# Softmax of the taps on every channel's own row, and two taps of the remaining channels mixed on TensorE, in a two-layer MoE kernel

## What is computed

```python
w = np.exp(weight - weight.max(-1, keepdims=True))          # weight: (8, 7)
w = w / (w.sum(-1, keepdims=True) + 1e-09)
out = np.einsum('hk,bskhg->bshg', w, x_unf)                 # x_unf: 7 shifted copies of x, zeros ahead
h = out @ w_in                                              # layer 1: 192 -> 2048
g = np.where(h >= 1, h, np.where(h <= -1, 0, (h + 1) ** 2 / 4))
x = g @ w_out                                               # 2048 -> 192
r = np.maximum(x @ w_in2, 0)                                # layer 2
return (s * r * r + b) @ w_out2
```

## Time and profile before

| | |
|---|---|
| median of three runs | 1127.93 us |
| the profiled execution's own time | 1127.12 us |
| its span in the profile | 1125.0 us |
| PE busy | 1117.5 us (99%) |
| DVE busy | 857.4 us (76%) |
| ACT busy | 692.0 us (62%) |
| POOL busy | 3.5 us |

### The profile page before, as it was taken

How to read it: one execution, slowest core, us unless ns; L and a number is a source line. 1 busy time by engine, 2 the same in 40 slices (tenths; PEclk the granted TensorE clock), 3 DMA queues, 4 the chain that set the end, 5 groups by cost and what they waited for, 6 DMA issues and landing times.

```text
span 1125.0 us, 22920 instructions
## 1 busy us (share of the span) xinstructions
PE 1117.5 (99%) x9756; PEld 981.5 (87%) x9756; DVE 857.4 (76%) x775; ACT 692.0 (62%) x690; POOL 3.5 (0%) x16
## 2 busy tenths in 40 slices
PE   8999999999999999999999999999999999999998
PEld 6888888888888888888888888888888888888887
DVE  7998888687787777877788677787777877666665
ACT  6977765576555756556655666556655566665544
POOL 1000000000000000000000000000000000000000
PEclk9999999999999999999999999999999999999999
DMA  5121100100000000010000100001000000000000
GB/s 159 30 67 52 44 1 1 29 29 1 1 1 29 29 1 1 1 29 29 1 1 1 40 18 1 1 11 47 1 1 1 1 29 1 1 1 1 29 1 29
DMA packets 13044, 21.30 MB, mean 19 GB/s; under 512 B 1184, under 2 KB 5792, under 8 KB 12960
## 3 DMA queue, kind: packets, MB, share of 16 engines
q1 hardware_dynamic: 12800, 19.86, 6.1%
q10 hardware_dynamic: 96, 0.13, 0.0%
q0 software_dynamic: 64, 0.00, 0.0%
HBM read 13.70 MB, written 6.29 MB: 18 GB/s over the span
## 4 chain that ended last, share of the span: by engine, by line
PE 98%; DVE 1%; DMA 0%; ACT 0%; issue 0%; ACTq 0%
PE h L821 31%; PE acc L868 30%; PE acc_rem L879 20%; PE h L834 15%; PE acc L1019 1%; DMA stage<-in_moe_w_out 0%; DVE mixed_rem L652 0%; PE h L1002 0%; PE acc L908 0%; ACT shared L540 0%; DVE g L558 0%; DVE up_lo L682 0%; ACT g_hi L370 0%; PE acc_rem L902 0%; DVE x_rem L752 0%
## 5 line engine op out<-in xcount | busy, mean ns | idle before, releaser
L561 DVE SCALAR_TENSOR_TENSOR g<-r,scale,h 128x1024 f32<-128x1024 f32 x128 | 161.8, 1277 | 95.1 <-ACT r L351 95.0
L372 ACT ACTIVATE g_hi<-g,shift 128x1024 fp32r<-128x1024 f32 x127 | 146.4, 1153 | 114.3 <-PE acc_rem L879 104.9
L348 ACT ACTIVATE r<-h,half 128x1024 f32<-128x1024 f32 x128 | 138.0, 1112 | 115.5 <-PE h L834 115.0
L351 ACT ACTIVATE r<-h 128x1024 f32<-128x1024 f32 x128 | 127.4, 1026 | 127.2 <-PE h L834 123.7
L821 PE MATMUL h<-x_rem,up_rem_hi 64*128 64x512 f32 x1016 | 204.7, 386 | 0.0
L868 PE MATMUL acc<-g_hi,dn_hi 64*128 64x512 f32 x1016 | 204.6, 386 | 0.0
L879 PE MATMUL acc_rem<-g_lo,dn_rem 64*128 64x512 f32 x1016 | 204.6, 386 | 0.0
L879 PE MATMUL acc_rem<-g_hi,dn_rem 64*128 64x512 f32 x1016 | 204.6, 386 | 0.0
L868 PE MATMUL acc<-g_lo,dn_hi 64*128 64x512 f32 x1016 | 204.6, 386 | 0.0
L868 PE MATMUL acc<-g_hi,dn_lo 64*128 64x512 f32 x1016 | 204.6, 386 | 0.0
L582 DVE SCALAR_TENSOR_TENSOR g_lo<-g,shift,g_hi 128x1024 fp32r<-128x1024 f32 x127 | 162.7, 1281 | 34.9 <-ACT g_hi L372 34.9
(11 more groups left out here) (152 smaller groups left out, 1406.9 us busy)
## 6 DMA issues: line engine op xcount, KB each, us to landing
xraw<-in_x SPq DMA_DIRECT2D x7, 518.0 KB, 4.2
out<-res SPq DMA_DIRECT2D x7, 512.0 KB, 3.3
stage<-in_moe_w_out SPq DMA_DIRECT2D x6, 384.0 KB, 3.3
xraw_rem<-in_x SPq DMA_DIRECT2D x14, 129.5 KB, 3.9
out<-res_rem SPq DMA_DIRECT2D x7, 256.0 KB, 3.7
stage<-in_moe_w_in SPq DMA_DIRECT2D x6, 256.0 KB, 5.8
stage<-in_moe_w_in SPq DMA_DIRECT2D x2, 512.0 KB, 4.7
xraw<-in_x SPq DMA_DIRECT2D x2, 256.0 KB, 2.9
```

The source lines that it names most:

```text
L348: nc.scalar.activation(r[k][:], h[k][:], ACT.Relu, scale=0.5, bias=half[:, 0:1]).then_inc(r_ready if two else relu_done[k], 1)
L351: nc.scalar.activation(r[k][:], h[k][:], ACT.Relu).then_inc(r_ready, 1)
L372: nc.scalar.activation(dst[:], g[k][:], ACT.Identity, bias=shift[:, 0:1]).then_inc(hi_ready, 1)
L561: nc.vector.scalar_tensor_tensor(g[k][:], r[k][:], scale[:, 0:1], h[k][:], ALU.mult, ALU.mult).then_inc(h_used, 1)
```

## The change

The 8-row load, the matrix `head_of` and the three spreading matmuls go. In their place:

- `head_rows` cuts the channels at head borders. ScalarE issues two transfers for the main part (120 rows and 8 rows), GpSimd four for the remaining part (16 and 48 rows, for each batch). The source repeats a head's row of 7 numbers for each of its channels, so every partition gets its own taps.
- The softmax works on 128 partitions. The maximum is negated and goes into the exponent as a bias. The sums are made by five small GpSimd instructions for each part, and inverted by VectorE. The scalar loads `scale` and `shift` on GpSimd now stand behind these.
- TensorE mixes taps 5 and 6 of the remaining part into `acc_rem` with two diagonal matrices (`diag_rem`, made by ScalarE in the upper half of `y_rem`); VectorE adds the result to `mixed_rem` in place of two taps of its own.
- TensorE opens with three `warm_up` matmuls instead of two.
- In block 0's first phase, ScalarE's pieces 8 to 10 and tap 0 of the main part move later, VectorE's `scale_taps` moves from ahead of slice 2 to ahead of slice 4, and piece 9 behind three taps.

The line numbers in the diff and in the rows of the new order are those of the changed kernel, about 20 to 32 higher.

```diff
-        head_taps = sb("head_taps", [HEADS, TAPS + 1])
-        tmax = sb("tmax", [HEADS, 1])
-        tsum = sb("tsum", [HEADS, 1])
-        head_of = sb("head_of", [HEADS, P + 2 * REM])
+        taps_in = sb("taps_in", [P, 2, TAPS])
+        tmax = sb("tmax", [P, 2])
+        tsum = sb("tsum", [P, 2])
+        three = sb("three", [P, 3])
...
+        diag_rem = y_rem[:, 2 * P:4 * P].rearrange("p (k c) -> p k c", c=P)
+        rem_pe = acc_rem[:, 0, :]
...
+        def head_rows(first, end):
+
+            c = first
+            while c < end:
+                head = c // GROUP
+                heads = (end - c) // GROUP if c % GROUP == 0 else 0
+                if heads:
+                    n = heads * GROUP
+                    src = weight[head:head + heads].unsqueeze(1).broadcast_to([heads, GROUP, TAPS])
+                else:
+                    n = min(GROUP - c % GROUP, end - c)
+                    src = weight[head].partition_broadcast(n)
+                yield c - first, c - first + n, src
+                c += n
+
+        MAIN_ROWS, REM_ROWS = list(head_rows(0, P)), list(head_rows(P, D))
+        PE_TAPS = 2
...
             sp.wait_ge(mixed_pe_done, 1)
-            sp.wait_ge(first_mix, 2 * TAPS - 1)
+            sp.wait_ge(first_mix, 2 * TAPS - PE_TAPS)
             load_x(1)
...
-            for cols, pattern, base in ((head_of[:, 0:P], [[1, P]], 0), (twice, [[0, 2], [1, REM]], P)):
-                for sign, off in ((1, base), (-1, GROUP - 1 - base)):
-                    pool.wait_ge(head_of_step, done)
...
             nc.gpsimd.memset(ident, 0.0).then_inc(ident_step, 1)
             pool.wait_ge(ident_step, 1)
             nc.gpsimd.affine_select(out=ident, in_=ident, compare_op=ALU.not_equal, fill=1.0, base=0,
...
+            for t in range(B):
+                for a, b_, src in REM_ROWS:
+                    pool.dma_start(taps_in[t * REM + a:t * REM + b_, 1, :], src).then_inc(rem_taps_loaded, 16)
             nc.gpsimd.memset(half[:], 0.5).then_inc(half_set, 1)
+            for part, ready in enumerate((main_taps_ready, rem_taps_ready)):
+                pool.wait_ge(ready, 1)
+                row, total = taps[:, part, :], tsum[:, part:part + 1]
+                nc.gpsimd.tensor_tensor(three[:], row[:, 0:3], row[:, 3:6], ALU.add).then_inc(sum_step, 1)
+                pool.wait_ge(sum_step, 5 * part + 1)
+                nc.gpsimd.tensor_tensor(total, three[:, 0:1], three[:, 1:2], ALU.add).then_inc(sum_step, 1)
+                pool.wait_ge(sum_step, 5 * part + 2)
+                nc.gpsimd.tensor_tensor(total, total, three[:, 2:3], ALU.add).then_inc(sum_step, 1)
+                pool.wait_ge(sum_step, 5 * part + 3)
+                nc.gpsimd.tensor_tensor(total, total, row[:, 6:7], ALU.add).then_inc(sum_step, 1)
+                pool.wait_ge(sum_step, 5 * part + 4)
+                nc.gpsimd.tensor_scalar(total, total, 1e-9, None, ALU.add).then_inc(sum_step, 1)
...
-            act.dma_start(head_taps[:, 0:TAPS], weight).then_inc(weight_loaded, 16)
-            act.wait_ge(taps_step, 2)
-            nc.scalar.activation(head_taps[:, 0:TAPS], head_taps[:, 0:TAPS], ACT.Exp).then_inc(taps_exp, 1)
-            act.wait_ge(taps_step, 6)
+            for a, b_, src in MAIN_ROWS:
+                act.dma_start(taps_in[a:b_, 0, :], src).then_inc(main_taps_loaded, 16)
+            act.wait_ge(main_max_ready, 2)
+            nc.scalar.activation(taps[:, 0, 0:TAPS], taps_in[:, 0, :], ACT.Exp, bias=tmax[:, 0:1]).then_inc(main_taps_ready, 1)
+            act.wait_ge(main_taps_ready, 1)
             act.wait_ge(ident_step, 2)
             for k in range(TAPS):
-                if k == 2:
-                    act.wait_ge(sums_spread, 1)
-                    nc.scalar.activation(taps[:, 1, :], spread_rem, ACT.Copy).then_inc(sums_ready, 1)
                 nc.scalar.activation(diag[:, k, :], ident, ACT.Copy, scale=taps[:, 0, k:k + 1]).then_inc(diag_done, 1)
-            act.wait_ge(sums_spread, 2)
-            nc.scalar.activation(taps[:, 0, TAPS:TAPS + 1], spread_sum, ACT.Copy).then_inc(sums_ready, 1)
-            act.wait_ge(sums_ready, 1)
+            weights_hi(0, 0)
+            act.wait_ge(rem_max_ready, 1)
+            nc.scalar.activation(tmax[:, 1:2], tmax[:, 1:2], ACT.Copy, scale=-1.0).then_inc(rem_max_ready, 1)
+            act.wait_ge(rem_max_ready, 2)
+            nc.scalar.activation(taps[:, 1, 0:TAPS], taps_in[:, 1, :], ACT.Exp, bias=tmax[:, 1:2]).then_inc(rem_taps_ready, 1)
+            act.wait_ge(rem_taps_ready, 1)
             act.wait_ge(x_rem_first_loaded, 32)
             act.wait_ge(halo_cleared, 2)
             nc.scalar.activation(mixed_rem[:], xraw_rem[:, 0:T], ACT.Copy,
                                  scale=taps[:, 1, 0:1]).then_inc(rem_tap0_done, 1)
-            weights_hi(0, 0)
+            for k in range(PE_TAPS):
+                tap = TAPS - PE_TAPS + k
+                nc.scalar.activation(diag_rem[:, k, :], ident, ACT.Copy,
+                                     scale=taps[:, 1, tap:tap + 1]).then_inc(diag_rem_done, 1)
             weights_hi(0, 1)
             act.wait_ge(first_mix, TAPS)
-            act.wait_ge(sums_ready, 2)
+            act.wait_ge(sums_ready, 1)
             nc.scalar.activation(X2[0][:, 0, :], mixed[:, 0, :], ACT.Copy,
                                  scale=taps[:, 0, TAPS:TAPS + 1]).then_inc(x_hi_done[0], 1)
             for n in (2, 3):
@@ -497,17 +526,17 @@
                                  scale=taps[:, 0, TAPS:TAPS + 1]).then_inc(mixed_pe_hi, 1)
             for n in (4, 5, 6):
                 weights_hi(0, n)
-            act.wait_ge(first_mix, 2 * TAPS - 1)
+            act.wait_ge(sums_ready, 2)
+            act.wait_ge(first_mix, 2 * TAPS - PE_TAPS)
             nc.scalar.activation(X2[2][:, 0, :], mixed_rem[:], ACT.Copy,
                                  scale=taps[:, 1, TAPS:TAPS + 1]).then_inc(x_rem_hi_done[0], 1)
             weights_hi(0, 7)
             act.wait_ge(half_set, 1)
...
-            e[1].append(lambda: weights_hi(0, 8))
             w = lambda n: lambda: weights_hi(0, n)
             phase(0, None, 0, 0, blk=0, extras=e,
-                  early={4: [w(9), lambda: tap0(0)], 6: [w(10), lambda: tap0(1)], 8: [w(11)],
+                  early={4: [w(8), lambda: tap0(0)], 6: [w(9), w(10)], 8: [w(11), lambda: tap0(1)],
...
-            dve.wait_ge(taps_step, 6)
+            dve.wait_ge(main_taps_loaded, 16 * len(MAIN_ROWS))
+            nc.vector.reduce_max(tmax[:, 0:1], taps_in[:, 0, :], AX.X).then_inc(main_max_ready, 1)
+            dve.wait_ge(main_max_ready, 1)
+            nc.vector.tensor_scalar(tmax[:, 0:1], tmax[:, 0:1], -1.0, None, ALU.mult).then_inc(main_max_ready, 1)
+            dve.wait_ge(main_taps_ready, 1)
             dve.wait_ge(halo_cleared, 2)
 
             for k in range(TAPS):
+                if k == 4:
+                    dve.wait_ge(rem_taps_loaded, 16 * B * len(REM_ROWS))
+                    nc.vector.reduce_max(tmax[:, 1:2], taps_in[:, 1, :], AX.X).then_inc(rem_max_ready, 1)
+                if k == TAPS - 1:
+                    dve.wait_ge(sum_step, 5)
+                    nc.vector.reciprocal(taps[:, 0, TAPS:TAPS + 1], tsum[:, 0:1]).then_inc(sums_ready, 1)
                 mix_first(k)
             weights_lo(0, 0)
...
-            for k in range(4, TAPS):
+            for k in range(4, TAPS - PE_TAPS):
                 mix_first_rem(k)
+            dve.wait_ge(sum_step, 10)
+            nc.vector.reciprocal(taps[:, 1, TAPS:TAPS + 1], tsum[:, 1:2]).then_inc(sums_ready, 1)
+            dve.wait_ge(first_mix, 2 * TAPS - PE_TAPS - 1)
+            dve.wait_ge(rem_pe_done, 1)
+            nc.vector.tensor_tensor(mixed_rem[:], rem_pe, mixed_rem[:], ALU.add).then_inc(first_mix, 1)
...
-            e = {2: [w(5), w(6), scale_taps],
-                 4: [w(7), w(8), m(0, 1)],
-                 6: [w(9), m(0, 2), m(0, 3), m(0, 4)],
+            e = {2: [w(5), w(6)],
+                 4: [scale_taps, w(7), w(8), m(0, 1)],
+                 6: [m(0, 2), m(0, 3), m(0, 4), w(9)],
...
             pe.wait_ge(warm_set, 1)
-            warm_up(2 * P)
-            warm_up(2 * P)
-            pe.wait_ge(taps_exp, 1)
-            pe.wait_ge(head_of_step, 5)
-            nc.tensor.matmul(spread_main, head_of[:, 0:P], head_taps[:, 0:TAPS], start=True, stop=True).then_inc(taps_spread, 1)
-            pe.wait_ge(taps_step, 5)
-            nc.tensor.matmul(spread_rem, head_of[:, P:], head_taps[:], start=True, stop=True).then_inc(sums_spread, 1)
-            nc.tensor.matmul(spread_sum, head_of[:, 0:P], head_taps[:, TAPS:TAPS + 1], start=True, stop=True).then_inc(sums_spread, 1)
-            pe.wait_ge(taps_step, 6)
-
+            for _ in range(3):
+                warm_up(2 * P)
             pe.wait_ge(x_first_loaded[1], 16)
             pe.wait_ge(halo_cleared, 2)
             for k in range(TAPS):
@@ -1019,6 +1043,13 @@
                 last = nc.tensor.matmul(mixed_pe, diag[:, k, :], xraw[:, 1, k:k + T],
```

(20 more changed lines are left out.)

31 lines of the change are left out of this document (11 added, 20 removed).

## The result

The changed kernel is slower. Its median is 1129.97 us (11 runs, 1128.63 to 1130.64) against 1127.51 (11 runs, 1126.65 to 1128.13) of the kernel before, run beside it: a ratio of 1.0021 with a 95% interval from 1.0011 to 1.0030. That is 2.5 us more, and no run of the one reaches the runs of the other. I had forecast 1.7 us less and a time of 1125.4, with 1128.0 as the upper end. The profiled execution took 1129.37 (span 1127.3), 2.25 above the one of before.

The account below looks back on a forecast made before the run. The time was taken as the moment TensorE's stream becomes dense plus a fixed length, only the first 32 us being changeable. An earlier first `r` (1.1) plus early slices (0.6) made 1.7 us: 1125.4, range 1124.3 to 1128.0.

Parts of the forecast that it names:

- When do the rows land?: ScalarE's head rows at the start: usable at 3.2 us, with bounds of 2.84 and 7.6; called the unknown.
- rival 4: ScalarE's rows land behind most of SyncE's queue, at 7.6: diagonals 8.6 to 16.4, time 1129.9; chance of slower 0.06.
- The start: ScalarE's table load ends near 3.37, the exponent at 3.6; VectorE starts at 3.63, 0.47 us earlier; TensorE's diagonals near 4.47.
- TensorE's diagonals and its clock: Clock rises to 2.4 GHz by 6.4 at the latest; diagonals end at about 11.6 instead of 12.5; new matmuls cost 1.72.
- VectorE up to the last rows of x: A stall of 0.5 us for GpSimd's transfers, landing at 7.0; taps end at 9.7, VectorE free at 12.8.
- The remaining part: VectorE's last tap, reciprocal and PSUM addition (0.7) end at 15.2, against 16.25; TensorE is nearly level.
- D: The advance of the moment ScalarE can form the first `r`, 18.42 before; forecast 1.1 us, set by VectorE.
- Slices 1 to 5: Moved jobs on ScalarE and VectorE remove waits, including TensorE's 0.47 for the `g` of slice 2: together 0.6 us.
- Rival 2: The 120 rows land late behind SyncE's loads, at 4.8; diagonals at 5.8; time 1126.3 to 1127.7; chance 0.18.

Follow-up runs that it names:

- e1_loads_wait: The changed kernel with SyncE's loads of x and weights starting only after ScalarE's two row transfers have landed; 1131.50 us (1 run).
- e2_ten_warm: The changed kernel with ten warm-up matmuls instead of three; median 1128.16 us, ratio 1.0009 to the kernel before.
- e12_one_head_wait: The changed kernel with one transfer of head 0's row to 128 partitions, and SyncE's loads waiting for the rows; 1129.03 us (1 run).
- e8_one_head: The changed kernel with ScalarE's two row transfers replaced by one repeating head 0's row on 128 partitions; median 1127.33 us, ratio 0.9999 to the kernel before.
- e5_ten_warm_again: The changed kernel with ten warm-up matmuls instead of three, run a second time; median 1128.17 us, ratio 1.0007 to the kernel before.
- e7_ten_warm_no_rem_pe: The changed kernel with ten warm-ups and no mixing of the remaining part's taps on TensorE; median 1128.89 us, ratio 1.0016 to the kernel before.

## Why the prediction was wrong

**When do the rows land?** This is the step that failed. I took 3.2 with bounds of 2.84 and 7.6; they were used at 6.24, and at 6.3 to 6.7 in the four traces of the same shape with ten warm-ups. Three terms were mis-sized, and together they make the 3.0 us. The second issue began at 2.12, not 1.43 (+0.7): I had the price of a transfer of 8 rows, 0.62, for one of 120, which took 1.39. On top of the lower bound I put 0.36, "a few rows of 9 ns each"; in e1_loads_wait, without traffic, it was 4.20 - (2.12 + 1.41) = 0.67 (+0.3), since all 128 pass as if one after another, 1.0 to 1.1, and only a part of that is over when the second transfer starts. And SyncE's traffic costs 2.0 (6.24 - 4.20) where I had counted nothing, because the request is made first; it is, but its packets start only at 2.8, a us behind SyncE's first. The argument against rival 4, that the 8 rows had been past the queue after 1.41, did not carry over to 128.

**The start.** That the table load would end near 3.4 assumed issues of 1.24 together; they took 1.77 and it ended at 3.81. The rows, later still, covered it.

**TensorE's diagonals and its clock.** I expected the rise by 6.4, since the third warm-up would reach nearly to the diagonals. It ended at 4.1 as planned; the diagonals came at 7.51. The mechanism, that a TensorE kept busy runs its diagonals sooner at 2.4 GHz, is what e2_ten_warm shows. I had priced the clock per us of an earlier rise and had not asked what 3.4 us of idleness do: 1.3 to 1.6 us. Nor were three warm-ups a safe number: in e12_one_head_wait the clock was up when the diagonals began, in the kernel after, e8_one_head and e1_loads_wait it was not.

**VectorE up to the last rows of x.** Its second reduction did not stall. GpSimd's transfers landed 3.8 to 4.5 us after their issue, later than the 3.4 I took, but VectorE itself was 3.2 later. With the rows at 4.23 the stall appears, 0.61 in e8_one_head. GpSimd's five small sums were done ahead of their reader.

**The remaining part.** The addition from PSUM took 0.69 (0.7 in the sum), the two matmuls 1.72 (1.72). But D was not set by VectorE in the kernel after. The diagonals' end, the two matmuls and `first_pair` are one unbroken chain on TensorE, 7.51 to 21.20. With the clock up VectorE is the bound, as I had it: in e5_ten_warm_again TensorE waits for its `x_rem` at 19.25. The mixing was worth 0.5 behind the diagonals with the 8-row softmax, and 0.7 in e7_ten_warm_no_rem_pe.

**Slices 1 to 5.** The trace pair gives the 0.6 (1106.6 to 1106.0 behind the first `r`), the repeats do not: 0.1 and less. TensorE's wait for the `g` of slice 2 is gone, as I had said, but it was not there in the repeat of the kernel before either. I was right that nobody is stopped for long; one new loss of 0.15 us is at slice 7, whose matmuls begin 1.51 behind those of slice 6 (1.36 before):

```profile
41.38 0.39 PE L853 MATMUL h<-x_hi,up_hi 64*128 64x512 f32 x2
...
42.89 0.50 PE L853 MATMUL h<-x_hi,up_hi 64*128 64x512 f32 x2
```

**The rivals.** Rival 2 named the right mechanism, and its chain was sound: it had the diagonals at 5.8 for rows at 4.8, and D down to -1.1; rows at 6.24 move that to 7.2 and -2.5, and measured were 7.51 and -2.87. Its landing, and so its price (1126.3 to 1127.7), was too low. Rival 4 has the time, 1129.9, with rows at 7.6, diagonals from 8.6 to 16.4 and D at -3.4; the rows came 1.4 earlier and the diagonals took 0.5 longer than it had, which gives 1129.37 in the profiled execution. That its 1129.9 stands next to the median of 1129.97 is luck. Both had chances too small for a transfer of which no row existed: my own bounds reached from 2.84 to 7.6, and I put the likeliest value less than a tenth of the way up.
